# Sequence passes and a mean moved between two parts of up products, in a fused Fourier and two-MLP kernel on one core

## The chip, the cores and the metric

The kernel runs on one core of one Trainium2 chip. The metric is the device time of one execution in microseconds (us); the median of several executions is used. Engines are named as in the profile: PE is TensorE, DVE is VectorE, ACT is ScalarE, POOL is GpSimd, SP is SyncE (here it only issues DMAs).

## The reference

```python
def _attn_ref(x):                                   # x: 2 x 3008 x 256
    return np.fft.fft(np.fft.fft(x, axis=1), axis=2).real.astype(np.float32)

def _moe_ref(x, w_gate, w_val, w_out, rms_g):       # 6016 tokens, 256 -> 1536 -> 256
    rms = np.sqrt(np.mean(x * x, axis=-1, keepdims=True) + 1e-06)
    xn = x / rms * rms_g
    g = xn @ w_gate
    return ((g / (1.0 + np.exp(-g))) * (xn @ w_val) @ w_out).astype(np.float32)

def _moe2_ref(x, w_in, w_out):                      # 256 -> 2048 -> 256
    h = x @ w_in
    return (h * np.cos(h) @ w_out).astype(np.float32)

def reference(...):                                 # everything in float32
    return _moe2_ref(_moe_ref(_attn_ref(x).reshape(6016, 256), ...), ...)
```

## The kernel before

All arrays are fp32. The Fourier transform is done as matrix products in stages, and both MLPs work on tiles of columns.

**First stage** (lines 455 to 481). The sequence of 3008 is split as 32 x 94. `x` comes in 11 chunks, DVE folds each (L886 to L896), and PE multiplies it with a table (L474 to L479). 24 row pairs `m` form 8 groups of 3 (`GROUPS`), each with two products `c` = 0 and 1, in one of four PSUM banks `(2 * g + c) % 4`. ACT copies each bank out (L658) and turns two rows of `c` = 1 (L666); DVE does this for `c` = 1 of the last group (L906, L912), which PE computes first in its group. PE then waits for all of it (L482).

**Second stage**, the loop over `G` = 0 to 33 (L530 to L538): `features(G)` (PE L492), `pq_copy(G)` (DVE L925), `sequence(G)` (PE L508, L510), `uv_copy(p)` for two steps at a time (ACT L678). `square(q)` (ACT L694), `add_squares(q)` (POOL L1122), `rms(q)` (PE L526) and `mean_copy(q)` (ACT L703) make the mean squares in nine parts; `spread_mean(q)` (SP L349) sends them into `stat`, and `root` (ACT L711), `recip` (DVE L932) and `inverse` (POOL) make 1/rms for three groups of rows. Beside it the weights of the first up product are scaled and mixed on DVE (`SCALE_AT`, `MIX_AT`: the step `G` after which each piece is done; L942, L956) and each is split into a high and a low part: `split_w1(n)` on ACT (L717, L720), then `w1_add(n)` (POOL L1104), a DMA that adds in its destination, 512 KB each, six of them. Pieces 4 and 5 are split inside the first tile.

**Tiles** (6 of 502 columns). A product `three(...)` is three matmuls (L541, L542, L543). For each of 12 blocks `i`, `up1(t, i)` makes two halves `m` (gate and value), each with a sum part and a dif part in two PSUM banks. DVE makes `plus` from the sum part (L995) and two tokens from `plus` and the dif part (L1003, L1004; `g_ready` for the gate half, `v_ready` for the value half). ACT does Silu (L806), POOL the product with the value (L1184, token 1 first), ACT `h_hi` (L767), and `h_lo` comes from DVE for token 0 (L980) and from POOL for token 1 (L1095). `down(t, i)` follows two blocks behind. The second MLP follows in the same tile.

Each engine's instructions run in the order in which they are written. The parts that the change touches are ordered by hand. In the first tile SP runs this list, in order (a few lines between them left out):

```python
            for q in STAT_MEANS[2][:-1]:
                spread_mean(q)
            sp.wait_ge(uv_done, LAST)
            load(wo2_raw[:, :], wo2, wo2_in)
...
            for n in range(W1_CHUNKS):
                sp.wait_ge(w1_lo_done[n], 16)
            load(win2_raw[:, :], win2, win2_in)
            spread_mean(MEANS - 1)
```

The last part of the mean can therefore be spread only after all six `w1_add` have landed and `win2` (2 MB) has been issued. ACT's `root(1)` and `root(2)` stand in block `i` = 5 of the first tile, ahead of `hi1` of block 5.

Of the kernel before, what the change touches and what calls it, by code (L numbers as in the profile page):

```python
# [76 lines left out]
def build(nc, x, w1a, w1b, small, wo1, win2, wo2, t_seq1, t_feat, t_seq2, t_const, out):  # L77
    ctx = ExitStack()
    with ctx:
# [5 lines left out]
        def sb(name, shape, at, dt=F32):  # L85
# [94 lines left out]
        raw_a_in, raw_b_in = ([sem(f"raw_{ab}_in{i}") for i in range(3)] for ab in "ab")  # L180
        even_done, odd_done, folded, n1_done, n1_main, n1_last, n1_out, seq1_turned = (sem(n) for n in (
            "even_done", "odd_done", "folded", "n1_done", "n1_main", "n1_last", "n1_out", "seq1_turned"))
        pq_done, pq_out, uv_done, uv_main = (sem(n) for n in ("pq_done", "pq_out", "uv_done", "uv_main"))
# [265 lines left out]
        def _(pe):  # L449
# [8 lines left out]
            for g, ms in enumerate(GROUPS):  # L458
                for i, m in enumerate(ms):
                    if m in CHUNK_AT:  # L460
                        if m:
                            warm_up(2 if CHUNK_AT.index(m) < 4 else 0)
                        pe.wait_ge(folded, CHUNK_AT.index(m) + 1)
                        if CHUNK_AT.index(m) == HALF_FOLDED[0]:
                            pe.wait_ge(seq1_turned, 4)
                    for c in group_order(g):
                        if i == 0 and g >= 2:
                            pe.wait_ge(n1_out, 3 * (g - 2) + 2 * c + 1)
                        if m == 0 and c:
                            pe.wait_ge(seq1_turned, 2)  # L470
                        acc = ps[:, (2 * g + c) % 4, i * COLS1:(i + 1) * COLS1]
# [68 lines left out]
            def three(acc, w_hi, w_lo, v_hi, v_lo, start, stop):  # L540
                nc.tensor.matmul(acc, w_hi, v_hi, start=start, stop=False)  # L541
                nc.tensor.matmul(acc, w_hi, v_lo, start=False, stop=False)  # L542
                return nc.tensor.matmul(acc, w_lo, v_hi, start=False, stop=stop)  # L543

            def up1(t, j, halves=(0, 1)):

                for m in halves:
                    if j:
                        pe.wait_ge(plus_done, 2 * (C1 * t + j - 1) + m + 1)
                    elif not (isinstance(t, int) and t == 0):  # L550
                        pe.wait_ge(cos_done, 2 * (C2 * t - 1 + m))
                    if isinstance(t, int) and t == 0 and j % 4 == 0:
                        pe.wait_ge(w1_lo_done[j // 2 + m], 16)
                    w = slice(m * FF1 + j * P, m * FF1 + (j + 1) * P)
                    three(ps[:, bank_pair(m), 0:N], sum_hi[:, w], sum_lo[:, w],
                          uv_hi[:, 0, 0:N], uv_lo[:, 0, 0:N], True, True)
                    if j:
                        pe.wait_ge(v_ready if m else g_ready, (C1 - m) * t + j)
                    three(ps[:, bank_pair(m) + 1, 0:N], dif_hi[:, w], dif_lo[:, w],
                          uv_hi[:, 1, 0:N], uv_lo[:, 1, 0:N], True, True).then_inc(up_done, 1)  # L560

# [35 lines left out]
            def tile(t, first=False):  # L597
                if not first:
# [9 lines left out]
                up1(t, 1, halves=(1,))  # L608
                if not first:
                    down(t - 1, ITEMS - 1, tokens=(1,))  # L610
                for i in range(2, C1):
                    up1(t, i, halves=(0,))
# [33 lines left out]
        def _(act):  # L646
# [8 lines left out]
            for g, ms in enumerate(GROUPS):  # L655
                for c in range(1 if g == NG - 1 else 2):
                    act.wait_ge(n1_done, 2 * g + group_order(g).index(c) + 1)
                    nc.scalar.activation(  # L658
                        g_sb[:, :, c, :, 2 * ms[0]:2 * ms[-1] + 2],
                        ps[:, (2 * g + c) % 4, 0:len(ms) * COLS1].rearrange(  # L660
                            "p (n b k) -> p b k n", b=BATCH, k=2 * K1), ACT.Copy
                        ).then_inc(n1_main if c else n1_out, 1)
                    if c:
                        act.wait_ge(n1_main, g + 1)
                        for part in range(2):
                            nc.scalar.activation(  # L666
                                g_sb[0:1, :, 1, part::2, 2 * ms[0]:2 * ms[-1] + 2],
                                ps[0:1, (2 * g + 1) % 4, 1 - part:len(ms) * COLS1:2].rearrange(
                                    "p (n b k) -> p b k n", b=BATCH, k=K1), ACT.Copy,
# [125 lines left out]
            def tile(t, first=False, last=False):  # L795
                for i in range(C1):
# [6 lines left out]
                    elif not first:  # L803
# [75 lines left out]
        def _(dve):  # L879
            nc.vector.memset(zeros[:, :], 0.0).then_inc(zeros_ready, 1)  # L880
            nc.vector.memset(stat[0:1, 0, 0:1], 1.0).then_inc(root_ready, 1)
            for i in range(XL):
# [20 lines left out]
            nc.vector.tensor_scalar(w128[:, :], sm[:, 3:], g128, None, ALU.mult).then_inc(g_done, 1)  # L903
            dve.wait_ge(n1_done, 2 * NG - 1)
            ms = GROUPS[-1]
            nc.vector.tensor_copy(  # L906
                g_sb[:, :, 1, :, 2 * ms[0]:2 * ms[-1] + 2],
                ps[:, (2 * NG - 1) % 4, 0:len(ms) * COLS1].rearrange("p (n b k) -> p b k n", b=BATCH, k=2 * K1)
                ).then_inc(n1_last, 1)
            dve.wait_ge(n1_last, 1)  # L910
            for part in range(2):
                nc.vector.tensor_scalar(  # L912
                    g_sb[0:1, :, 1, part::2, 2 * ms[0]:2 * ms[-1] + 2],
                    ps[0:1, (2 * NG - 1) % 4, 1 - part:len(ms) * COLS1:2].rearrange(
                        "p (n b k) -> p b k n", b=BATCH, k=K1),
                    1.0 if part else -1.0, None, ALU.mult).then_inc(n1_out, 1)
            dve.wait_ge(g_done, 3)
# [175 lines left out]
        def _(pool):  # L1093
# [85 lines left out]
            def tile(t, first=False, last=False):  # L1179
                for i in range(C1 - 1):  # L1180
# [96 lines left out]
```

## Time and profile before

| what | value |
|---|---|
| median of 3 runs | 984.19 us (983.29 to 986.62) |
| the profiled execution: time | 984.3 us |
| the profiled execution: span, first to last instruction | 982.5 us |
| PE busy | 972.3 us (99% of the span) |
| DVE, ACT, POOL busy | 742.9, 638.7, 350.4 us |
| PE's waits for DVE at L541 (in tiles), together | 1.5 us (0.6 + 0.5 + 0.4) |
| granted PE clock | 1.000 of full |

The times of the text are microseconds from the start of the span. What lies around the span is 984.3 - 982.5 = 1.8 us. A matmul's duration in the profile is longer than the distance to the next, since they are pipelined: distances between starts are what counts on PE.

### The profile page before, as it was taken

Reading aid. Unit: us, or ns where it says so; the run is one execution under the profiler, and the core shown is the slowest. Engines: PE = TensorE matmul, PEld = TensorE weight load, DVE = VectorE, ACT = ScalarE, POOL = GpSimd, SP = SyncE. Lnnn points to the kernel's source line nnn. Section 1 sums busy time; section 2 is a strip of 40 time slices with the busy share of each in tenths; the row PEclk is TensorE's granted clock in tenths of the full one; section 3 lists DMA queues with packets and bytes.
Section 4 is the critical chain, followed back from the end, with each engine's and each line's share of the span. In section 5 each row is a group of like instructions: output and inputs, shape, how many; then the busy total and the mean of one; then the engine's idle time right before and its main releaser. Section 6 shows DMA issues by size and latency. Waiting matters only on the chain.

```text
span 982.5 us, 13009 instructions
## 1 busy us (share of the span) xinstructions
PE 972.3 (99%) x4518; PEld 807.9 (82%) x4518; DVE 742.9 (76%) x1028; ACT 638.7 (65%) x803; POOL 350.4 (36%) x292
## 2 busy tenths in 40 slices
PE   8999999999999999999999999999999999999998
PEld 8978788888888888888888888888888888888886
DVE  6887987768876768877667877767887767887665
ACT  5586778764468774458775448776448776437777
POOL 0377874027730007750007751005661004770000
PEclk9999999999999999999999999999999999999999
DMA  9788002001010001010001010001000000000001
GB/s 332 235 221 235 1 1 53 0 1 43 1 43 1 1 0 42 0 40 2 0 0 42 0 32 11 0 0 42 0 32 0 0 0 7 36 0 0 0 0 42
DMA packets 14082, 36.80 MB, mean 37 GB/s; under 512 B 2618, under 2 KB 6682, under 8 KB 13658
## 3 DMA queue, kind: packets, MB, share of 16 engines
q1 hardware_dynamic: 11978, 31.63, 9.4%
q0 software_dynamic: 2064, 4.72, 2.7%
q8 instruction: 15, 0.25, 0.1%
q14 instruction: 25, 0.20, 0.1%
HBM read 22.35 MB, written 9.26 MB: 32 GB/s over the span
## 4 chain that ended last, share of the span: by engine, by line
PE 91%; DMA 3%; POOL 2%; DVE 2%; issue 1%; ACT 1%; SPq 0%; DVEq 0%; ACTq 0%; POOLq 0%
PE ps L541 30%; PE ps L543 30%; PE ps L542 30%; DMA x_sb<-x 1%; POOL work L1184 1%; PE ps L492 1%; DMA stat<-mean_row 1%; DMA w_lo<-w_f 1%; PE ps L510 1%; PE ps L508 0%; SPq L319 0%; POOL squares L1122 0%; POOL uv_t L1141 0%; POOL w_lo L1104 0%; POOL h_lo L1095 0%
## 5 line engine op out<-in xcount | busy, mean ns | idle before, releaser
L541 PE MATMUL ps<-h_hi,wo_hi 128*128 128x502 f32 x672 | 261.5, 389 | 0.6 <-DVE h_lo L980 0.6
L543 PE MATMUL ps<-h_hi,wo_lo 128*128 128x502 f32 x672 | 261.3, 389 | 0.0
L542 PE MATMUL ps<-h_lo,wo_hi 128*128 128x502 f32 x672 | 261.1, 389 | 0.0
L1095 POOL TENSOR_TENSOR h_lo<-work,h_hi 128x502 fp32r<-128x502 f32 x92 | 101.5, 1111 | 373.8 <-ACT h_hi L782 369.9
L767 ACT ACTIVATE h_hi<-work 128x502 fp32r<-128x502 f32 x132 | 82.4, 626 | 174.2 <-POOL work L1184 173.9
L1082 DVE SCALAR_TENSOR_TENSOR work<-work,ps 128x1004 f32<-128x1004 f32 (+1 forms) x109 | 117.2, 1075 | 95.6 <-ACT work L864 95.2
L1068 DVE SCALAR_TENSOR_TENSOR work<-work,ps 128x1004 f32<-128x1004 f32 (+1 forms) x109 | 116.5, 1074 | 48.0 <-ACT work L850 47.9
L541 PE MATMUL ps<-x_hi,win_hi 128*128 128x502 f32 x384 | 150.0, 391 | 0.0
L541 PEld LDWEIGHTS ps<-h_hi,wo_hi 128*128 128x128 f32 x672 | 126.2, 188 | 28.2 <-issue 0.8
L542 PE MATMUL ps<-x_lo,win_hi 128*128 128x502 f32 x384 | 149.3, 389 | 0.0
L543 PE MATMUL ps<-x_hi,win_lo 128*128 128x502 f32 x384 | 149.2, 389 | 0.0
L543 PEld LDWEIGHTS ps<-h_hi,wo_lo 128*128 128x128 f32 x672 | 126.3, 188 | 25.9
L542 PEld LDWEIGHTS ps<-h_lo,wo_hi 128*128 128x128 f32 x672 | 126.3, 188 | 25.9
L995 DVE SCALAR_TENSOR_TENSOR plus<-u,w,ps 128x502 f32<-128x502 f32 x144 | 105.8, 735 | 50.6 <-PE ps L543 49.8
L850 ACT ACTIVATE work<-ps 128x1004 f32<-128x1004 f32 (+1 forms) x109 | 98.2, 907 | 60.1 <-PE ps L543 59.3
L859 ACT ACTIVATE work<-work 128x1004 f32<-128x1004 f32 (+1 forms) x109 | 102.7, 942 | 31.1 <-DVE work L1068 30.3
L1184 POOL TENSOR_TENSOR work<-work,uv_t 128x502 f32<-128x502 f32 x72 | 99.1, 1398 | 46.6 <-DVE uv_t L1004 44.8
L988 DVE TENSOR_TENSOR h_lo<-work,h_hi 128x502 fp32r<-128x502 f32 x172 | 114.3, 703 | 1.3
L541 PE MATMUL ps<-uv_hi,w_hi 128*128 128x502 f32 x288 | 112.8, 392 | 0.9 <-DVE work L1004 0.5
L542 PE MATMUL ps<-uv_lo,w_hi 128*128 128x502 f32 x288 | 112.0, 389 | 0.0
L543 PE MATMUL ps<-uv_hi,w_lo 128*128 128x502 f32 x288 | 111.9, 389 | 0.0
L782 ACT ACTIVATE h_hi<-work 128x1004 fp32r<-128x1004 f32 (+1 forms) x109 | 101.7, 939 | 14.8 <-PE ps L543 8.7
(89 smaller groups left out, 1275.7 us busy)
## 6 DMA issues: line engine op xcount, KB each, us to landing
out<-y_sb SPq DMA_DIRECT2D x10, 502.0 KB, 3.0
x_sb<-x SPq DMA_DIRECT2D x6, 768.0 KB, 10.3
w_lo<-w_f POOLq DMA_DIRECT2D x6, 512.0 KB, 7.0
uv_t<-uv_dram SPq DMA_DIRECT2D x6, 502.0 KB, 3.5
wo_raw<-wo SPq DMA_DIRECT2D x1, 2048.0 KB, 8.5
win_raw<-win SPq DMA_DIRECT2D x1, 2048.0 KB, 9.4
raw_b<-w1b SPq DMA_DIRECT2D x3, 512.0 KB, 12.4
raw_a<-w1a SPq DMA_DIRECT2D x3, 512.0 KB, 12.3
```

The source lines that it names most:

```text
L541: nc.tensor.matmul(acc, w_hi, v_hi, start=start, stop=False)
L542: nc.tensor.matmul(acc, w_hi, v_lo, start=False, stop=False)
L543: return nc.tensor.matmul(acc, w_lo, v_hi, start=False, stop=stop)
L782: nc.scalar.activation(h_hi[j % 2][:, gs, 0:N], work[j % 4][:, gs, :], ACT.Copy).then_inc(hi_done, gs.stop - gs.start)
L850: nc.scalar.activation(work[j % 4][:, gs, :], ps[:, bank_pair(j) + gs.start:bank_pair(j) + gs.stop, 0:N], ACT.Copy, bias=MAGIC).then_inc(r ...
L859: nc.scalar.activation(work[j % 4][:, gs, :], work[j % 4][:, gs, :], ACT.Sin, scale=TURN / 2).then_inc(sin_done, gs.stop - gs.start)
L988: nc.vector.tensor_tensor(h_lo[j % 2][:, g, 0:N], work[j % 4][:, g, :], h_hi[j % 2][:, g, 0:N].bitcast(F32), ALU.subtract).then_inc(hid_sp ...
L995: nc.vector.scalar_tensor_tensor(out=plus[m][:, :], in0=u128[:, :], scalar=w128[:, m * C1 + i:m * C1 + i + 1], in1=ps[:, bank_pair(m), 0:N ...
L1068: nc.vector.scalar_tensor_tensor(out=buf, in0=buf, scalar=MAGIC, in1=pair, op0=ALU.subtract, op1=ALU.subtract).then_inc(frac_done, gs.stop ...
L1082: nc.vector.scalar_tensor_tensor(out=buf, in0=buf, scalar=1.0, in1=pair, op0=ALU.subtract, op1=ALU.mult).then_inc(cos_done, gs.stop - gs.s ...
L1095: nc.gpsimd.tensor_tensor(dst, src, hi.bitcast(F32), ALU.subtract).then_inc(s, 1)
L1184: nc.gpsimd.tensor_tensor(work[i % 3][:, g, :], work[i % 3][:, g, :], value[i % 2][:, g, :], ALU.mult).then_inc(h_done[g], 1)
```

## The change

- First stage: six PSUM banks instead of four; the last group of three row pairs becomes a group of two and a group of one. DVE copies out `c` = 1 of both, with a semaphore of its own (`n1_turned`).
- `sequence(32)` and `sequence(33)` move from between the halves of `up1(0, 0)` to between the sum and dif parts of the halves of `up1(0, 1)`; `rms(7)` (the eighth mean) moves to between the sum and dif parts of `up1(0, 2)`'s first half. The last `uv_copy` on ACT moves behind the first Silu.
- `rms(6)` moves from step 32 to step 33. `square(8)` and `add_squares(8)` move from block 0 to block 1 of the first tile.
- The second `plus` buffer lies elsewhere, since `pq` is still read when it is first written.
- `w1_add(2)` moves ahead of `add_squares(5)` on POOL.
- The mixings of all weight pieces but the last are done by step 24, and the scalings by step 21.
- `down(0, 0)` takes token 1 first, and waits for the eighth mean's copy ahead of both tokens.

```diff
-        plus = [sb(f"plus{i}", [N], o_pq + i * TB // 2) for i in range(2)]
+        plus = [sb("plus0", [N], o_pq), sb("plus1", [N], o_x2 + 1024)]
-        GROUPS = [range(i, i + 3) for i in range(0, H // 2, 3)]
+        GROUPS = [range(i, i + 3) for i in range(0, H // 2 - 3, 3)] + [range(H // 2 - 3, H // 2 - 1), range(H // 2 - 1, H // 2)]
+        def n1_bank(g, c):
+            return (2 * g + c) % 6
         def group_order(g):
-            return (1, 0) if g == NG - 1 else (0, 1)
+            return (1, 0) if g >= NG - 2 else (0, 1)
-        RMS_AT = [8, 9, 15, 20, 24, 28, 32]
+        RMS_AT = [8, 9, 15, 20, 24, 28, 33]
-        SCALE_AT = [2, 6, 10, 19, 23, 28]
-        MIX_AT = [3, 5, 8, 9, 16, 18, 20, 22, 24, 26, 31, 32]
+        SCALE_AT = [2, 6, 10, 16, 20, 21]
+        MIX_AT = [3, 5, 8, 9, 11, 13, 18, 19, 23, 24, 31, 32]
-                        if i == 0 and g >= 2:
-                            pe.wait_ge(n1_out, 3 * (g - 2) + 2 * c + 1)
+                        if i == 0 and g >= 3:
+                            pe.wait_ge(n1_out, 3 * (g - 3) + 2 * c + 1)
-            pe.wait_ge(n1_out, 3 * NG)
+            pe.wait_ge(n1_out, 3 * NG - 4)
+            pe.wait_ge(n1_turned, 4)
...
-                up1(t, 1, halves=(0,))
                 if first:
+                    up1_sum(t, 1, 0)
+                    sequence(LAST - 2)
+                    up1_dif(t, 1, 0)
+                    up1_sum(t, 1, 1)
+                    sequence(LAST - 1)
+                    up1_dif(t, 1, 1)
+                    up1_sum(t, 2, 0)
                     rms(RMS_LATE[0])
+                    up1_dif(t, 2, 0)
                 else:
+                    up1(t, 1, halves=(0,))
                     down(t - 1, ITEMS - 1, tokens=(0,))
...
-                        down(t, 0, tokens=(0,))
                         pe.wait_ge(mean_out, MEANS - 1)
-                        down(t, 0, tokens=(1,))
+                        down(t, 0, tokens=(1, 0))
...
             up1(0, 0, halves=(0,))
-            sequence(LAST - 2)
-            sequence(LAST - 1)
+            pe.wait_ge(pq_out, LAST)
             pe.wait_ge(mean_out, len(RMS_AT))
             up1(0, 0, halves=(1,))
...
-            for p in range(LAST // 2):
+            for p in range(LAST // 2 - 1):
...
                     if first and i == 0:
+                        uv_copy(LAST // 2 - 1)
+                        mean_copy(RMS_LATE[0])
+                    if first and i == 1:
                         square(MEANS - 1)
-                        mean_copy(RMS_LATE[0])
...
             w1_add(1)
+            w1_add(2)
             add_squares(5)
             scale_uv(0)
             scale_u128(0)
-            w1_add(2)
             add_squares(6)
...
-                    if first and i == 0:
+                    if first and i == 1:
                         add_squares(MEANS - 1)
```

`up1` is otherwise cut into `up1_sum` and `up1_dif` with the same waits and matmuls, and DVE's copy of the last group becomes a loop over the last two groups.

## Rows read from the trace of the kernel before

**Rows 1.** Windows: busy us (instructions) of PE, PEld, DVE, ACT, POOL, then clock, DMA share, GB/s.
```profile
76.00:88.00 12.00, 12.00 (x62) 9.62 (x61) 9.51 (x16) 9.58 (x14) 10.84 (x11) 1.00 0.98 213
...
200.00:300.00 100.00, 100.00 (x443) 82.71 (x442) 78.59 (x117) 55.94 (x76) 51.43 (x41) 1.00 0.06 21
```
**Rows 2.** PE's waits in the whole span: total us, times, longest.
```profile
PE ps L526 <- POOL squares L1122: 1.3, 1, 1.3
...
PE ps L492 <- DVE g_sb L912: 0.9, 1, 0.9
PE ps L541 <- DVE h_lo L980: 0.6, 2, 0.4
```
**Rows 3.** The chain that ended last, 78 to 110: start, us, what.
```profile
78.28 7.38 DMA w_lo<-w_f
...
85.73 0.35 SPq L319
...
86.98 9.03 DMA stat<-mean_row
...
96.12 0.04 ACT stat L711
...
109.81 0.49 PE ps L541
```
**Rows 4.** Timeline, 24 to 26: start, duration, what.
```profile
24.56 0.58 DVE L906 COPY g_sb<-ps 128x408 f32<-128x408 f32 x1 [1.13 <-PE ps L475]
...
25.18 0.63 DVE L912 TENSOR_SCALAR g_sb<-ps 1x204 f32<-1x204 f32 x2
...
25.87 1.56 PE L492 MATMUL ps<-feat,g_sb 128*96 128x129 f32 x12 [0.88 <-DVE g_sb L912]
```
**Rows 5.** Timeline, 55 to 60.
```profile
55.20 0.81 ACT L694 ACTIVATE squares<-uv 128x752 f32<-128x752 f32 x1
55.33 1.21 DVE L935 TENSOR_TENSOR uv_lo<-uv_t,uv_hi 128x1004 fp32r<-128x1004 f32 x1 [0.25 <-ACT uv_hi L744]
...
56.15 1.29 POOL L1122 TENSOR_TENSOR squares<-squares 128x376 f32<-128x376 f32 x1
...
57.93 0.47 DVE L925 SCALAR_TENSOR_TENSOR pq<-feat,ps 96x256 f32<-96x256 f32 x1
...
59.18 0.47 PE L541 MATMUL ps<-uv_hi,w_hi 128*128 128x502 f32 x1
...
59.67 0.47 DVE L925 SCALAR_TENSOR_TENSOR pq<-feat,ps 96x256 f32<-96x256 f32 x1
```
**Rows 6.** ACT's timeline, 64 to 72.
```profile
64.73 0.98 ACT L694 ACTIVATE squares<-uv 128x940 f32<-128x940 f32 x1
65.61 0.22 ACT L703 ACTIVATE mean_row<-ps 128x94 f32<-128x94 f32 x1
66.69 0.62 ACT L767 ACTIVATE h_hi<-work 128x502 fp32r<-128x502 f32 x1 [0.85 <-POOL work L1184]
...
71.53 0.63 ACT L767 ACTIVATE h_hi<-work 128x502 fp32r<-128x502 f32 x1
```
**Rows 7.** POOL's timeline, 65 to 74.
```profile
65.33 2.49 POOL L1184 TENSOR_TENSOR work<-work,uv_t 128x502 f32<-128x502 f32 x2 [1.81 <-DVE uv_t L1004]
...
68.82 1.00 POOL L1122 TENSOR_TENSOR squares<-squares 128x470 f32<-128x470 f32 x1
...
72.68 1.08 POOL L1095 TENSOR_TENSOR h_lo<-work,h_hi 128x502 fp32r<-128x502 f32 x1
73.70 1.20 POOL L1104 DMA_DIRECT2D w_lo<-w_f  x1
```
**Rows 8.** DVE's and POOL's timelines: the same DVE instruction with and without POOL beside it.
```profile
74.25 0.68 DVE L980 TENSOR_TENSOR h_lo<-work,h_hi 128x502 fp32r<-128x502 f32 x1
...
114.31 1.25 DVE L980 TENSOR_TENSOR h_lo<-work,h_hi 128x502 fp32r<-128x502 f32 x1
...
113.72 1.30 POOL L1095 TENSOR_TENSOR win_lo<-win_raw,win_hi 128x512 fp32r<-128x512 f32 x1
```

More of the change, by code:

```diff
@@ L154, in build @@
         zeros = sb("zeros", [P], o_pq)
-        plus = [sb(f"plus{i}", [N], o_pq + i * TB // 2) for i in range(2)]
+        plus = [sb("plus0", [N], o_pq), sb("plus1", [N], o_x2 + 1024)]
+        assert o_work + 4 * GCOLS <= o_x2 + 1024 and o_x2 + 1024 + 4 * N <= o_hid - UVB
         o_end = o_pq + pad(max(TB, 16 * DIM))
@@ L180, in build @@
         raw_a_in, raw_b_in = ([sem(f"raw_{ab}_in{i}") for i in range(3)] for ab in "ab")
-        even_done, odd_done, folded, n1_done, n1_main, n1_last, n1_out, seq1_turned = (sem(n) for n in (
-            "even_done", "odd_done", "folded", "n1_done", "n1_main", "n1_last", "n1_out", "seq1_turned"))
+        even_done, odd_done, folded, n1_done, n1_main, n1_last, n1_turned, n1_out, seq1_turned = (sem(n) for n in (
+            "even_done", "odd_done", "folded", "n1_done", "n1_main", "n1_last", "n1_turned", "n1_out", "seq1_turned"))
         pq_done, pq_out, uv_done, uv_main = (sem(n) for n in ("pq_done", "pq_out", "uv_done", "uv_main"))
@@ L543, in three, with up1_sum, up1_dif @@
                 return nc.tensor.matmul(acc, w_lo, v_hi, start=False, stop=stop)
+            def up1_sum(t, j, m):
+                if j:
+                    pe.wait_ge(plus_done, 2 * (C1 * t + j - 1) + m + 1)
+                elif not (isinstance(t, int) and t == 0):
+                    pe.wait_ge(cos_done, 2 * (C2 * t - 1 + m))
+                if isinstance(t, int) and t == 0 and j % 4 == 0:
+                    pe.wait_ge(w1_lo_done[j // 2 + m], 16)
+                w = slice(m * FF1 + j * P, m * FF1 + (j + 1) * P)
+                three(ps[:, bank_pair(m), 0:N], sum_hi[:, w], sum_lo[:, w],
+                      uv_hi[:, 0, 0:N], uv_lo[:, 0, 0:N], True, True)
+            def up1_dif(t, j, m):
+                w = slice(m * FF1 + j * P, m * FF1 + (j + 1) * P)
+                if j:
+                    pe.wait_ge(v_ready if m else g_ready, (C1 - m) * t + j)
+                three(ps[:, bank_pair(m) + 1, 0:N], dif_hi[:, w], dif_lo[:, w],
+                      uv_hi[:, 1, 0:N], uv_lo[:, 1, 0:N], True, True).then_inc(up_done, 1)
             def up1(t, j, halves=(0, 1)):
                 for m in halves:
[L548 to L560, printed above, removed]
+                    up1_sum(t, j, m)
+                    up1_dif(t, j, m)
             def up2(t, j):
@@ L602, in tile @@
                     up1(t, 0, halves=(1,))
-                up1(t, 1, halves=(0,))
                 if first:
+                    up1_sum(t, 1, 0)
[5 more added lines that the diff above has]
+                    up1_sum(t, 2, 0)
                     rms(RMS_LATE[0])
+                    up1_dif(t, 2, 0)
                 else:
+                    up1(t, 1, halves=(0,))
                     down(t - 1, ITEMS - 1, tokens=(0,))
-                up1(t, 1, halves=(1,))
-                if not first:
+                    up1(t, 1, halves=(1,))
                     down(t - 1, ITEMS - 1, tokens=(1,))
+                    up1(t, 2, halves=(0,))
                 for i in range(2, C1):
-                    up1(t, i, halves=(0,))
+                    if i > 2:
+                        up1(t, i, halves=(0,))
                     if first and i == LAST_MEAN_AT + 1:
@@ L655, in _ @@
             for g, ms in enumerate(GROUPS):
-                for c in range(1 if g == NG - 1 else 2):
+                for c in range(1 if g >= NG - 2 else 2):
                     act.wait_ge(n1_done, 2 * g + group_order(g).index(c) + 1)
@@ L659, in _ @@
                         g_sb[:, :, c, :, 2 * ms[0]:2 * ms[-1] + 2],
-                        ps[:, (2 * g + c) % 4, 0:len(ms) * COLS1].rearrange(
+                        ps[:, n1_bank(g, c), 0:len(ms) * COLS1].rearrange(
                             "p (n b k) -> p b k n", b=BATCH, k=2 * K1), ACT.Copy
@@ L667, in _ @@
                                 g_sb[0:1, :, 1, part::2, 2 * ms[0]:2 * ms[-1] + 2],
-                                ps[0:1, (2 * g + 1) % 4, 1 - part:len(ms) * COLS1:2].rearrange(
+                                ps[0:1, n1_bank(g, 1), 1 - part:len(ms) * COLS1:2].rearrange(
                                     "p (n b k) -> p b k n", b=BATCH, k=K1), ACT.Copy,
@@ L903, in _ @@
             nc.vector.tensor_scalar(w128[:, :], sm[:, 3:], g128, None, ALU.mult).then_inc(g_done, 1)
[L904 to L916, printed above, removed]
+            for g in (NG - 2, NG - 1):
+                ms, bank = GROUPS[g], n1_bank(g, 1)
+                dve.wait_ge(n1_done, 2 * g + 1)
+                nc.vector.tensor_copy(
+                    g_sb[:, :, 1, :, 2 * ms[0]:2 * ms[-1] + 2],
+                    ps[:, bank, 0:len(ms) * COLS1].rearrange("p (n b k) -> p b k n", b=BATCH, k=2 * K1)
+                    ).then_inc(n1_last, 1)
+                dve.wait_ge(n1_last, g - NG + 3)
+                for part in range(2):
+                    nc.vector.tensor_scalar(
+                        g_sb[0:1, :, 1, part::2, 2 * ms[0]:2 * ms[-1] + 2],
+                        ps[0:1, bank, 1 - part:len(ms) * COLS1:2].rearrange(
+                            "p (n b k) -> p b k n", b=BATCH, k=K1),
+                        1.0 if part else -1.0, None, ALU.mult).then_inc(n1_turned, 1)
             dve.wait_ge(g_done, 3)
```

2 lines of the change are left out of this document (1 added, 1 removed).

## The prediction

> **What bounds the kernel now.** The windows come first: from 200 to 300 us, and in every window after it up to 960, PE is busy all the time at a granted clock of 1.00, the 2.4 GHz level [rows 1], and the change adds no PE work, so a gain or a loss can only come from the stretch before, where PE waits. PE's waits name the places: 1.3 us on POOL's squares ahead of `rms(6)`, 0.9 us on DVE's last copy of the first stage, 0.6 us on `h_lo` in two pieces, at `down(0, 0)` and, near 98 us, at `down(0, 5)` [rows 2]. I then read the chain that ended last, and it decides the case. Read it backwards from 109.81, where PE's last wait of the head ends: to `root(2)` on ACT at 96.12; to the DMA of the ninth mean into `stat`, issued at 86.98 and 9.03 us on its way; to the load of `win2` just ahead of it on SP's queue, at 85.73; to the last of the six weight adds, `w1_add(5)`, issued by POOL at 78.28 and landed after 7.38 us [rows 3]. SP's list says why: `win2` waits for all six. From 109.81 on PE doesn't wait for anything that matters. So the end of the kernel moves by as much as `w1_add(5)` moves, if its landing and what follows last as long as now. What PE gains before 78 us is not yet a gain: it arrives earlier at `down(0, 5)` and waits there longer.
>
> **First stage.** Before, the tail behind the last product is one copy of 408 columns (0.58 us) and two turns of 204 (0.63 together), and PE starts at 25.87 [rows 4]. After, the tail is 136 columns and turns of 68. By those two rows (0.58 for 408, 0.31 for 204: 0.0013 us a column) these take 0.22 and twice 0.14, 0.50 in all. The larger group's tail (272 columns 0.40, turns of 136 0.45) runs on DVE's idle time of 1.13 us before [rows 4], but can begin only some 0.75 before L906 did, at 23.8, and ends at 24.7, 0.15 after the last product. 25.87 - (24.7 + 0.5 + 0.05) is 0.6; small copies rarely come out as cheap as a line through two rows says, so I take 0.35, with bounds 0 and 0.6. The six banks cost nothing and by themselves give nothing: no row shows PE waiting for ACT's copies; they keep the group of one from waiting for a bank. Steps 0 to 31 are paced by PE, so the 0.35 goes through to everything at 56 us. Times below leave it out, and it comes into the sum at the end.
>
> **`rms(6)` a step later, `w1_add(2)` earlier.** PE loses 1.3 us at 57.55 [rows 2]. `features(33)` and `sequence(30)` (0.9 us, half of the steady 0.87 each and the switch) now run in it. Does `add_squares(6)` also come earlier, with the DMA issue gone ahead of it? Its input `square(6)` ends at 56.01 (55.20 + 0.81), and DVE's `uv_lo`, which reads two operands from SBUF, runs to 56.54 [rows 5]. DVE's `h_lo` takes 0.68 us alone and 1.25 when it is issued at 114.31, inside POOL's instruction from 113.72 to 115.02: it ends 0.54 after POOL [rows 8]. So the one waits for the other: the squares, 0.85 us by themselves (1.29 less what `uv_lo` holds them), still end at 57.4, and `rms(6)` starts at 57.5; if they did not wait it would be 57.0. The Trainium skill, SBUF — State Buffer, "SBUF: two separate sides", calls the port pair of the two engines an exclusive lock that the first holds for its whole instruction when DVE reads two inputs from SBUF; that too would give 57.5, and this trace agrees with 1.25 against 0.68 us. PE gains 0.9 of the 1.3. `w1_add(2)` fits into the wait that POOL had before `add_squares(5)` (2.6 us) and costs nothing. The mixings go to steps where DVE waits for PE; two stay at steps 31 and 32.
>
> **Into the tile.** DVE is next. `up1(0, 0)` waits for `pq_copy(32)`, which ends at 57.93 + 0.47 = 58.40 [rows 5]: it starts at 58.45, against 59.18 before, 0.73 earlier. The other half waits for `pq_copy(33)`, 60.14, which is a new wait of 0.3 on PE. DVE then runs through `plus` and tokens without a wait, since two sequence passes (0.8 us) no longer stand between. The first value is ready, and POOL's first product starts, at 64.4 against 65.33 [rows 7]: 0.94 earlier. PE's own gain at `down(0, 0)` comes to 1.45, as its three waits on DVE there shrink too.
>
> **What is queued behind the moved passes.** ACT now does `uv_copy(16)` and `mean_copy(7)` behind the first Silu, ahead of `hi1(0)`. PE reaches `rms(7)` after `up1(0, 0)` second half (60.2 + 1.44), two sums and two difs at 0.68 each with a switch (3.0), two sequence passes (0.84) and one more sum (0.68): 66.1. The copy follows half a us later, and `h_hi` starts at 66.75, against 66.69 [rows 6], although the product was ready at 65.65. The gain of 0.94 is gone for token 1 of block 0. ACT's second Silu comes 0.6 earlier than before; `square(8)`, 0.88 in distance [rows 6], now stands behind it, then the two splits: `h_hi` of block 1 at 71.7 against 71.53 [rows 6].
> POOL's `h_lo` of block 1 then runs at 72.4 against 72.68 (there it waited for the product), and behind it comes the moved `add_squares(8)` of 1.0 us [rows 7], ahead of `w1_add(4)`. DVE's `h_lo` (0.68) waits for the same lock since 73.0 and may go first: another 0.55. `w1_add(4)` goes out at 73.4 + 1.0 = 74.4, or 74.95, against 73.70 [rows 7]: 0.7 or 1.25 later. The squares are no new work, but before they ran from 68.82, and there POOL would now wait for ACT's Silu (until 68.9) anyway. From `w1_add(4)` to `w1_add(5)` is 78.28 - 73.70 = 4.58, one product, one `h_lo` and the issue, as before.
>
> **The sum.** `w1_add(5)` moves by +0.7 to +1.25 less the first stage's 0.35: +0.35 to +0.9. I take +0.6, the middle, since nothing tells which of the two gets the lock. The chain behind it is unchanged. The profiled execution took 984.3; 984.3 + 0.6 = 984.9. The median shown is 0.1 under the profiled execution: 984.8.
>
> **Free edits.** The second `plus` buffer's home: written and read by DVE alone as before; in `x2_hi`, which ACT writes only after the last token of the first MLP is made. Token 1 first in `down(0, 0)`: POOL's `h_lo` (68.4) is there before DVE's (69.1), PE arrives at 69.05, so it hides a wait of 0.1 to 1 us, which is PE's time and is given back at 98 us. The loop over tiles 1 to 5 keeps its order. A new wait: `up1(0, 4)`'s second half waits for the ninth mean's copy, on ACT behind the fourth Silu, perhaps 0.7 us; PE's again, and covered by the same later wait.
>
> **Rivals.**
> *POOL runs through early (22%).* If `rms(7)` and the squares cost POOL nothing, all of its list from 65.33 to 78.28, in which it never idles, moves by 0.94 + 0.35 = 1.3 earlier: 983.0 in the profiled execution, 982.9. It needs `rms(7)` half a us or more before my 66.1 and products faster than in rows 7. For it: POOL's total work there is the same. Against: ACT's order, worked out above.
> *PE's gain stays (7%).* If the chain over `win2` had slack that I don't see, PE keeps 0.35 + 1.45 and part of the late waits: 984.3 - 1.8 - 0.7, near 981.7. Against: the chain is unbroken from 78.28 to 109.81 [rows 3].
> *Slower: the transfers slip (13%).* SP spreads the eighth mean before it issues `wo2` (2 MB) and the 1.4 MB of `uv`. That mean is copied 1.0 later, 0.65 with the first stage, and the DMA engines are 98% busy in 76 to 88 [rows 1]. If the backlog moves by the full 0.65, the adds 4 and 5 land behind it: with the upper 0.9 for their issue and a first stage that gives nothing (0.35), 0.65 + 0.9 + 0.35 = 1.9: 986.1. It decides once `w1_add(5)` lands later than 87. The Trainium skill, DMA: Bandwidth & Descriptors, "Queues, rings and completion order", has a semaphore increment land only after every earlier write of that DMA engine, across its queues: a reason why a mean of 1.5 KB needs 9.03 us [rows 3], and the adds would wait for late stores in the same way.
> *As forecast (58%):* 984.1 to 985.6, no difference that can be told.
>
> **Range and chances.** About 0.3% (3 us) is what a measurement can tell here. 982.7 to 986.5 holds the forecast, most of the early rival, and most of the late one; outside lie the kept gain, and single mishaps. All of PE's waits that could go are 0.9 + 1.3 [rows 2] and the 1.5 in the tiles (the table above), 3.7 us, so over 0.3% faster needs nearly all of them: 4%. Over 0.3% slower needs the late rival and a us more: 4%. Within: 92%.
>
> **What the new profile would show.** PE's first feature matmul at 25.5; PE's wait for the squares under 0.5 us and a new one ahead of the second half of `up1(0, 0)`; POOL's first product at about 64; `mean_row`'s copy at 66.3 just ahead of `h_hi`; `w1_add(4)` at 74.1 to 74.6 and `w1_add(5)` at 78.6 to 79.2; `root(2)` at 96.5 to 97; and PE's wait for `h_lo` near 98, 0.2 before, grown to 1.5 or more. The prediction is wrong if `w1_add(5)` is issued before 78, if its landing or that of the mean isn't near 7.4 and 9.0, or if PE no longer waits at 98.

## The result and the profile after

The changed kernel takes 987.26 us (median of 21, 985.61 to 992.3), the kernel before 984.96 us (median of 21, 983.29 to 988.9): ratio 1.0028, interval 1.0017 to 1.0039. It is slower by 2.3 us in the medians and 2.8 by the ratio, just under the 0.3% that I had called the limit of what can be told, and outside my range. The profiled execution took 986.18 us, its span 984.2 us: it was one of the faster ones, 0.9 us under the median of the 13 executions at a mean granted clock of 1.00 (987.08), so the profile shows less of the loss than the times do.

PE's waits of the changed kernel, in total us, times, longest (`rms` is now L531, a product L546 to L548, `h_lo` on DVE L1001):

```profile
PE ps L546 <- DVE h_lo L1001: 1.5, 1, 1.5
PE ps L531 <- issue: 1.5, 1, 1.5
...
PE ps L546 <- ACT mean_row L721: 0.8, 1, 0.8
PE ps L497 <- ACT g_sb L676: 0.5, 1, 0.5
```

Against [rows 2]: the wait of 1.3 us for the seventh mean's squares is gone, and 1.5 us stand at another mean. The wait for `h_lo` has grown from 0.2 near 98 us (0.6 in two pieces) to 1.5, and the ninth mean's copy costs 0.8. The chain that ended last (start, us, what), the counterpart of [rows 3]:

```profile
79.72 6.88 DMA w_lo<-w_f
86.67 0.35 SPq L323
...
88.29 9.42 DMA stat<-mean_row
...
98.11 0.62 ACT h_hi L785 x2
...
111.51 0.50 PE ps L546
```

It is the same chain, 1.70 us later where PE leaves it (111.51 against 109.81), and the span is 1.7 us longer. The sixth weight add goes out 1.44 later (79.72 against 78.28); its landing is 0.5 quicker; from the load of `win2` to `root(2)` it is 0.75 longer (86.67 to 97.81, against 85.73 to 96.12).

Where the new wait comes from is seen on POOL, DVE and PE of the changed kernel (timelines; L1143 is `add_squares`, L1125 `w1_add`, L1150 to L1156 `inverse(0)`, L977 a mixing, L963 a scaling, L953 the reciprocal):

```profile
38.01 1.28 POOL L1143 TENSOR_TENSOR squares<-squares 128x376 f32<-128x376 f32 x1 [3.88 <-ACT squares L712]
39.24 2.92 POOL L1125 DMA_DIRECT2D w_lo<-w_f  x1
40.98 1.26 POOL L1150 TENSOR_TENSOR stat<-stat 6x94 f32<-6x94 f32 x1
42.31 0.48 POOL L1152 TENSOR_TENSOR stat<-stat 6x94 f32<-6x94 f32 x1
42.89 1.48 POOL L1154 TENSOR_SCALAR stat<-stat 6x94 f32<-6x94 f32 x1
44.45 0.86 POOL L1156 TENSOR_TENSOR stat<-stat 6x94 f32<-6x94 f32 x1
45.27 1.48 POOL L1143 TENSOR_TENSOR squares<-squares 128x376 f32<-128x376 f32 x2
...
38.57 1.28 DVE L977 SCALAR_TENSOR_TENSOR w_f<-raw_a,gvec,raw_b 128x512 f32<-128x512 f32 x1
...
40.16 0.72 DVE L953 RECIPROCAL stat<-stat 6x94 f32<-6x94 f32 x1
...
45.42 1.62 DVE L963 TENSOR_SCALAR raw_b<-raw_b,gvec 128x512 f32<-128x512 f32 x1
...
44.33 0.39 PE L515 MATMUL ps<-seq,pq 96*128 96x94 f32 x2
46.21 0.37 PE L531 MATMUL ps<-squares,consts 128*32 128x94 f32 x8 [1.50 <-issue]
```

The mixing at step 13 (0.74 by itself) and POOL's squares (0.84 in the kernel before) meet and take 1.28 each. The reciprocal of step 14 and `inverse(0)` follow late, and each small operation of `inverse(0)` is longer too (1.26, 0.48, 1.48 and 0.86 us, against 1.01, 0.34, 0.72 and 0.34 before). The squares of the fourth mean, next on POOL, start only at 45.27 (before: 42.81), and PE waits for them from 44.7 to 46.21.

### The profile page after: what moved, and what is told of

It reads as the page before. It is cut to its first block, busy times and chain, and to the rows that moved or that the text cites. A ratio compares the mean times of both kernels' runs of the same rounds, so it can differ in the third digit from the quotient of the medians.

```text
span 984.2 us, 13014 instructions
## 1 busy us (share of the span) xinstructions
PE 972.4 (99%) x4518; PEld 808.9 (82%) x4518; DVE 743.5 (76%) x1031; ACT 638.6 (65%) x804; POOL 352.5 (36%) x292
## 4 chain that ended last, share of the span: by engine, by line
PE 93%; DMA 3%; DVE 1%; ACT 1%; POOL 1%; issue 1%; SPq 0%; DVEq 0%; ACTq 0%
PE ps L546 30%; PE ps L547 30%; PE ps L548 30%; PE ps L497 2%; DMA x_sb<-x 1%; DMA stat<-mean_row 1%; PE ps L515 1%; DMA w_lo<-w_f 1%; PE ps L513 1%; POOL work L1205 0%; SPq L323 0%; ACT h_hi L785 0%; DVE x_sb L906 0%; PE ps L482 0%; PE ps L531 0%
## 5 line engine op out<-in xcount | busy, mean ns | idle before, releaser
L546 PE MATMUL ps<-h_hi,wo_hi 128*128 128x502 f32 x672 | 261.7, 389 | 1.5 <-DVE h_lo L1001 1.5
L548 PE MATMUL ps<-h_hi,wo_lo 128*128 128x502 f32 x672 | 261.6, 389 | 0.0
L546 PE MATMUL ps<-x_hi,win_hi 128*128 128x502 f32 x384 | 150.2, 391 | 0.0
L546 PEld LDWEIGHTS ps<-h_hi,wo_hi 128*128 128x128 f32 x672 | 126.3, 188 | 28.5 <-DVE h_lo L1001 2.2
L548 PE MATMUL ps<-x_hi,win_lo 128*128 128x502 f32 x384 | 149.4, 389 | 0.0
L548 PEld LDWEIGHTS ps<-h_hi,wo_lo 128*128 128x128 f32 x672 | 126.4, 188 | 25.8
L546 PE MATMUL ps<-uv_hi,w_hi 128*128 128x502 f32 x288 | 113.0, 392 | 1.5 <-ACT mean_row L721 0.8
L548 PE MATMUL ps<-uv_hi,w_lo 128*128 128x502 f32 x288 | 112.1, 389 | 0.0
## 6 DMA issues: line engine op xcount, KB each, us to landing
x_sb<-x SPq DMA_DIRECT2D x6, 768.0 KB, 10.4
```

## The experiments

Each was measured beside the kernel before. "Add 5 of 6" and "6 of 6" are the issue of the last two `w1_add`, and `root(2)` and the end of the span are given from PE's first feature matmul, since the loading of `x` shifts that by about 1 us between executions of like kernels (25.87 to 26.86 with the old first stage, 24.93 to 26.21 with the new). What the first stage itself gives is therefore not in these columns. "Early" is a `root(2)` that runs right behind `root(1)`, before 92.4 in the span.

| kernel | ratio (95%) | add 5, 6 of 6 | root(2) | span end |
|---|---|---|---|---|
| before | 1 | 47.83, 52.41 | 70.25 | 956.63 |
| changed | 1.0028 (1.0017 to 1.0039) | 49.76, 54.07 | 72.16 | 958.55 |
| a1 old mix steps | 1.0029 (1.0015 to 1.0042) | 52.05, 56.36 | 74.44 | 960.87 |
| a2 only mix steps | 1.0024 (1.0014 to 1.0035) | 49.15, 53.71 | 71.44 | 957.89 |
| a3 one mix moved back | 1.0017 (1.0009 to 1.0026) | 49.23, 53.52 | 71.75 | 958.23 |
| a4 mean before win2 | 0.9996 (0.9985 to 1.0007) | 49.85, 54.15 | early | 955.99 |
| b1 mixings apart | 1.0011 (1.0002 to 1.0020) | 49.12, 53.43 | 71.65 | 958.06 |
| b2 before, mean first | 0.9998 (0.9984 to 1.0013) | 47.86, 52.43 | early | 955.84 |
| b3 apart, mean first | 0.9992 (0.9982 to 1.0003) | 49.13, 53.43 | early | 955.24 |
| b4 apart, squares back | 0.9996 (0.9987 to 1.0005) | 46.86, 51.15 | 69.26 | 955.72 |
| c1 changed again | 1.0038 (1.0024 to 1.0051) | 51.75, 56.04 | 74.12 | 960.49 |
| c2 apart, squares back, mean first | 0.9971 (0.9961 to 0.9982) | 47.73, 52.02 | early | 953.94 |
| c3 also scaling early | 0.9973 (0.9963 to 0.9984) | 47.75, 52.04 | early | 954.03 |
| c4 before, squares later | 1.0025 (1.0015 to 1.0034) | 49.49, 53.80 | 71.98 | 958.35 |
| d1 changed, squares back | 1.0013 (1.0001 to 1.0025) | 50.35, 54.66 | 72.98 | 959.34 |
| d2 before, squares later, mean first | 0.9999 (0.9989 to 1.0008) | 49.48, 53.80 | early | 955.66 |

The first two rows are the two kernels of the first series. In every kernel in which the mean comes after `win2`, the end of the span less `root(2)` is 886.4 us (886.36 to 886.48). A kernel in which `root(2)` comes 1.7 later ends 1.7 later. With the mean first, `root(2)` no longer waits, and the end is PE's own.

**a1: the old steps for scaling and mixing, in the changed kernel.**

```diff
-        SCALE_AT = [2, 6, 10, 16, 20, 21]
-        MIX_AT = [3, 5, 8, 9, 11, 13, 18, 19, 23, 24, 31, 32]
+        SCALE_AT = [2, 6, 10, 19, 23, 28]
+        MIX_AT = [3, 5, 8, 9, 16, 18, 20, 22, 24, 26, 31, 32]
```

> The changed kernel with the scaling and mixing steps of before; all else as changed. Theory A (mixings at steps 11 to 19 stand beside POOL's squares and inverse(0), so that the squares for the fourth mean come late, PE waits 1.5 us at 44.7, and POOL's list carries it to the last weight add): the wait at 44.7 is gone, the last weight add is issued at 78.2 to 79.0 instead of 79.7, and the ratio to before falls from 1.0028 to 0.9995 to 1.0010. Theory B (what I predicted: the moved squares and ACT's order behind the moved passes are the cost, the mixings are free): the ratio stays at 1.002 to 1.003.

Measured 1.0029, outside theory A's range and inside theory B's; the last add goes out at 81.29 in the span, later than theory A had it. The wait at 44.7 is gone, and another of 2.2 us is there, from 52.7 to 54.89. Timelines of DVE and POOL, and windows of all engines (busy us of PE, PEld, DVE, ACT, POOL, then granted clock, DMA share, GB/s), of this kernel:

```profile
50.12 4.32 DVE L977 SCALAR_TENSOR_TENSOR w_f<-raw_a,gvec,raw_b 128x512 f32<-128x512 f32 x1
...
49.40 1.05 POOL L1143 TENSOR_TENSOR squares<-squares 128x376 f32<-128x376 f32 x1
50.22 2.47 POOL L1162 TENSOR_TENSOR uv_t<-uv_t,inv_t 128x502 f32<-128x502 f32 x2
52.45 1.43 POOL L1167 TENSOR_TENSOR u<-u,inv_t 128x502 f32<-128x502 f32 x1
```

The windows:

```profile
53.00:54.00 1.00, 0.00 (x0) 0.00 (x0) 1.00 (x1) 1.00 (x2) 0.88 (x1) 1.00 1.14 211
...
56.00:57.00 1.00, 1.00 (x7) 1.00 (x6) 0.41 (x2) 0.62 (x2) 0.40 (x1) 0.50 0.93 346
57.00:58.00 1.00, 1.00 (x6) 1.00 (x6) 1.00 (x2) 0.00 (x0) 0.00 (x0) 0.50 1.10 240
```

The mixing of step 26 is issued at 50.12, while POOL's squares run; three POOL products follow these without a gap, to 53.88, and the mixing ends at 54.44, 0.56 after them: it ran only when POOL had nothing more. The same place in the kernel before:

```profile
50.37 0.84 POOL L1122 TENSOR_TENSOR squares<-squares 128x376 f32<-128x376 f32 x1 [2.61 <-ACT squares L694]
51.19 3.04 POOL L1141 TENSOR_TENSOR uv_t<-uv_t,inv_t 128x502 f32<-128x502 f32 x2
...
51.09 0.74 DVE L956 SCALAR_TENSOR_TENSOR w_f<-raw_a,gvec,raw_b 128x512 f32<-128x512 f32 x1
```

Here the mixing was issued 0.1 before the end of the same squares, ran between them and the first product, and took 0.74, while the two products took 3.04 instead of 2.47. Counted from the first feature matmul, the mixing is issued at the same time in both (25.19 and 25.22), and POOL's operations follow each other without a gap in both. What differs is that in a1 the squares stand right behind the issue of the moved `w1_add(2)` and end 0.2 later (25.52 against 25.34). That this made the mixing lose its turn is likely, but no run shows it by itself. Either way the old steps are no longer free once the rest of the change is there: undoing this part alone exchanges one collision for another, so the ratio of 1.0029 is no support for theory B.

PE is idle during its wait, and then its granted clock is 0.50 for some 3 us, of which more under c1. Of a1's seven executions four have a mean granted clock of 0.998; the three at 1.00 have a median of 985.37, 1.0 us over before's 984.39, so much of a1's ratio is the clock.

**a2: the new steps alone, in the kernel before** (the diff of a1 the other way).

> The kernel before with the new scaling and mixing steps alone. Theory A: a wait of PE of about 1 to 1.5 us appears near 44.9, and the kernel is slower than before by 1 to 2.5 us, ratio 1.0010 to 1.0025. Theory B: ratio 0.9995 to 1.0005, no new wait.

Measured 1.0024, two waits of PE for squares, 2.5 us together, the longer one 1.5: theory A. That the mixings cost nothing, as I had it, is refuted.

**a3: one mixing from step 13 to 16, in the changed kernel.**

```diff
-        MIX_AT = [3, 5, 8, 9, 11, 13, 18, 19, 23, 24, 31, 32]
+        MIX_AT = [3, 5, 8, 9, 11, 16, 18, 19, 23, 24, 31, 32]
```

> The changed kernel with one single mixing moved, from step 13 to step 16 (where before had one); the others stay at the new steps. Theory A in its narrow form (the mixing at step 13, 38.6, delays the reciprocal at step 14 and the second weight piece, and these inverse(0) on POOL): reciprocal at 39.1 instead of 40.2, PE's wait at 44.7 under 0.6 us, ratio to before 0.9998 to 1.0015. Theory A in its wide form (all of the early mixings together): the wait stays over 1 us and the ratio over 1.0018. Theory B: no change from 1.0028.

Measured 1.0017. The wait for the fourth mean is gone and the reciprocal starts at 39.42: the narrow form, as far as the wait goes. The ratio lies between the two forms (1.0015 at most, over 1.0018), and its interval takes in both.

**a4: the last mean spread before `win2`, in the changed kernel.**

```diff
+            spread_mean(MEANS - 1)
             for n in range(W1_CHUNKS):
                 sp.wait_ge(w1_lo_done[n], 16)
             load(win2_raw[:, :], win2, win2_in)
-            spread_mean(MEANS - 1)
```

> The changed kernel with SP's order changed: the last mean is spread before the wait for the six weight adds and the load of win2, instead of behind it. Theory A2 (the end of the head is set by the chain last weight add, win2, last mean, root on ACT): root(2) comes at about 91 instead of 97.8, PE's wait of 1.5 us for h_lo near 100 goes, and the time falls by 1.5 to 2.5 us from the changed kernel, ratio to before 1.0000 to 1.0012. Rival (PE's time lost at 44.7 is lost for good and the late chain only hides it): the ratio stays over 1.0022.

Measured 0.9996, a little better than forecast: the loss is gone, with PE's wait of 1.5 us near 44.7 still in place. The late chain does set the end, as predicted.

**b1: mixings apart, in the changed kernel.**

```diff
-        SCALE_AT = [2, 6, 10, 16, 20, 21]
-        MIX_AT = [3, 5, 8, 9, 11, 13, 18, 19, 23, 24, 31, 32]
+        SCALE_AT = [2, 6, 10, 19, 21, 28]
+        MIX_AT = [3, 5, 8, 9, 16, 18, 20, 22, 23, 24, 31, 32]
```

> The changed kernel with mixings at 16, 18, 20, 22, 23, 24 (four of them where before had them) and scalings at 19, 21, 28: none stands beside inverse(0) at steps 11 to 15, and all but the last pair are done before POOL's unbroken run of uv and u128 products from 50. Theory A, as the first four runs leave it (it is the meeting of one DVE mixing with POOL's two-input instructions that costs, in either of two places): no wait of PE at 44 to 46 and no mixing over 1.7 us, last weight add issued at 78.3 to 79.2, root(2) at 96.3 to 97.2, ratio to before 1.0000 to 1.0010. Rival (the rest of the change, the squares and ACT's order in the first tile, carries most of the loss): last weight add after 79.4, ratio over 1.0015.

Measured 1.0011, just over the forecast and under the rival's 1.0015. POOL of this kernel, against the fence of the changed one above:

```profile
38.20 0.85 POOL L1143 TENSOR_TENSOR squares<-squares 128x376 f32<-128x376 f32 x1 [3.88 <-ACT squares L712]
38.99 2.05 POOL L1125 DMA_DIRECT2D w_lo<-w_f  x1
40.10 1.02 POOL L1150 TENSOR_TENSOR stat<-stat 6x94 f32<-6x94 f32 x1
...
41.63 0.72 POOL L1154 TENSOR_SCALAR stat<-stat 6x94 f32<-6x94 f32 x1
...
42.75 0.84 POOL L1143 TENSOR_TENSOR squares<-squares 128x376 f32<-128x376 f32 x1
```

The squares are back at 0.85 us and those of the fourth mean 2.5 us earlier. Add 6 of 6 is at 79.27 in the span, just over the forecast of this run, `root(2)` at 97.49, 0.3 over it. One collision is left: the scaling of step 28, issued at 52.76 beside the products that a1 showed, takes 2.34 us, where others take 0.47.

**b2, b3: the mean first, in the kernel before and in b1's.** The edit is that of a4.

> The kernel before with the last mean spread ahead of the wait for the weight adds and of win2. Theory A2 (the late chain sets the end of before too, by as much as PE waits at 98 and 107 to 110, 0.9 us in all): root(2) before 92, those waits gone, ratio to before 0.9988 to 0.9996. Rival (the chain was not binding in before): ratio 0.9997 to 1.0003.

> Both edits in the changed kernel: mixings apart, and the last mean ahead of win2. If PE's gain in the first tile is real and only hidden by the late chain, it now shows: 0.2 from the first stage, about 1 us from rms(6) and the passes, 0.9 from the late waits: ratio to before 0.9975 to 0.9988, the fastest of all. If the moved passes give PE nothing, ratio 0.9990 to 1.0000, as the kernel before with the mean first.

Measured 0.9998 and 0.9992. From the first feature the span is 0.8 and 1.4 us shorter than before, as expected of b2 and at the low end of b3, and the medians say the same (983.83 and 983.05 against 984.58). But both ratios lie in the ranges of the rivals, and their intervals reach into both ranges, so the times settle neither.

**b4: b1 with the squares back in block 0.**

```diff
                     if first and i == 0:
                         uv_copy(LAST // 2 - 1)
+                        square(MEANS - 1)
                         mean_copy(RMS_LATE[0])
-                    if first and i == 1:
-                        square(MEANS - 1)
...
-                    if first and i == 1:
+                    if first and i == 0:
                         add_squares(MEANS - 1)
```

> As the run with the mixings apart, but square(8) and add_squares(8) back in block 0 of the first tile, where before had them. My predicted mechanism (the squares of 1 us, and up to 0.55 of DVE's, ahead of the fifth weight add): the fifth weight add goes out 0.5 to 1.2 us earlier than with the mixings apart alone, and the ratio falls by 0.0005 to 0.0012. Rival (ACT, not POOL's squares, paces block 1: in block 0 square(8) stands in the time in which ACT waits for the eighth mean, but add_squares then delays POOL's next product): under 0.3 us of change.

Measured 0.9996 against 1.0011 of b1 (same chip, same runs of before). Add 5 of 6 goes out 2.26 us earlier, more than the 0.5 to 1.2 expected: not only the squares, but ACT's `square(8)` leaves block 1.

**c1: the changed kernel again.**

> The changed kernel itself once more, beside the kernel before on one chip, as a control for the three next to it. Theory A: the same profile as the first one, PE's wait of 1.5 us ahead of the fourth mean, ratio 1.002 to 1.003; and if the longer wait is what sometimes brings PE's granted clock down for some us, more of its executions than of before show a mean clock of 0.998. Rival (the gap to the mixings-apart run came from the chip and not from the wait): ratio 1.001 to 1.0015 here, and no difference in the clocks.

Measured 1.0038, over the forecast of 1.002 to 1.003. Three of five executions are at a mean granted clock of 0.998 (7 of 21 in the first series; the kernel before 3 of 21 beside c1, none of 11 in b1 and in b4, none of 8 in c2). This time the profiled one was among them. Its windows, columns as above:

```profile
44.00:46.00 2.00, 1.07 (x10) 0.91 (x9) 2.00 (x5) 1.11 (x3) 1.92 (x3) 1.00 1.03 177
46.00:47.00 1.00, 0.43 (x9) 0.32 (x10) 1.00 (x1) 0.00 (x0) 1.00 (x2) 1.00 0.12 21
47.00:48.00 1.00, 1.00 (x7) 1.00 (x8) 0.64 (x2) 0.00 (x0) 0.97 (x2) 0.62 0.62 60
48.00:49.00 1.00, 1.00 (x7) 1.00 (x7) 0.64 (x2) 0.38 (x1) 0.00 (x0) 0.50 0.84 275
49.00:50.00 1.00, 1.00 (x7) 1.00 (x7) 0.48 (x1) 1.00 (x3) 0.00 (x0) 0.50 1.04 308
50.00:51.00 1.00, 1.00 (x8) 1.00 (x8) 0.04 (x1) 0.97 (x2) 0.00 (x0) 0.68 0.93 141
51.00:52.00 1.00, 1.00 (x11) 1.00 (x10) 1.00 (x2) 0.81 (x3) 0.42 (x1) 1.00 1.13 228
```

PE stands still for 1.5 us in 44 to 47. Then the granted clock goes from 1.00 (2.4 GHz) to 0.50 (1.2 GHz), and is back at 1.00 from 51 on. The windows' clocks lack 0.38 + 0.5 + 0.5 + 0.32 = 1.7 us of full clock, and POOL's first product comes 1.8 us later after the first feature than in the first profile of the same kernel (41.45 against 39.63). The profiles of a1 and d1, which have 2.2 and 1.5 us of wait in front, show the same. The first profile of the changed kernel and that of a2 have the same wait of 1.5 us and no fall.

**c2, c3: what the change can give.** c2 is b4's kernel with a4's edit. c3 also has `SCALE_AT = [2, 6, 10, 17, 19, 21]`.

> Mixings apart, squares back in block 0, and the last mean spread ahead of win2: what PE gains in the first tile can no longer be hidden by the late chain. If the moved passes and the rms step are worth what PE's timeline says, ratio 0.9978 to 0.9990; if another chain takes over (the landing of win2 or the second MLP's weights), a new wait of PE after 100 us and a ratio of 0.9990 or more.

> As the run before, with the scalings at 17, 19, 21 instead of 19, 21, 28: the one at step 28 took 2.35 us instead of 0.47 beside POOL's unbroken run of products in the run with the mean first. It should take 0.47 again, features and sequences of steps 28 to 31 lose their 0.2 to 0.5 us of waits, and the time falls by 0.2 to 0.6 us more; the cost, if one is seen, is a backlog of DVE of up to 1 us at steps 22 to 24, which PE has two steps of slack for.

Measured 0.9971 and 0.9973, 981.84 and 981.87 us against 984.45: faster than both kernels. What is left of PE's waits in c2 after the first stage:

```profile
PE ps L531 <- issue: 0.3, 1, 0.3
PE ps L546 <- DVE work L1024: 0.2, 1, 0.2
PE ps L497 <- DVE pq L945: 0.2, 1, 0.2
```

Both are better than the forecast of c2. c3's further 0.2 to 0.6 us did not come: its waits for squares are 0.7 us, in two, instead of 0.3. The new one is again at the fourth mean, where the last operation of `inverse(0)` on POOL takes 1.64 us instead of 0.34.

**c4: the squares alone, in block 1 of the kernel before** (b4's edit the other way).

> The kernel before with one edit of the change alone: square(8) and add_squares(8) in block 1 instead of block 0. My predicted mechanism: the fifth and the sixth weight add go out 0.7 to 1.3 us later, root(2) with them, ratio 1.0007 to 1.0015. Rival (in the kernel before POOL would use the freed time of block 0, so the move is neutral there): the adds move by under 0.3 us, ratio 0.9997 to 1.0003.

Measured 1.0025, more than expected: 2.2 us by the executions at a granted clock of 1.00, 1.7 in the profile. POOL and ACT of this kernel, the counterpart of [rows 6, 7]:

```profile
73.20 1.08 POOL L1096 TENSOR_TENSOR h_lo<-work,h_hi 128x502 fp32r<-128x502 f32 x1 [0.87 <-ACT h_hi L767]
74.24 1.46 POOL L1123 TENSOR_TENSOR squares<-squares 128x470 f32<-128x470 f32 x1
75.64 1.20 POOL L1105 DMA_DIRECT2D w_lo<-w_f  x1
...
69.60 0.97 ACT L694 ACTIVATE squares<-uv 128x940 f32<-128x940 f32 x1
70.48 1.05 ACT L717 ACTIVATE w_hi<-w_f 128x1024 fp32r<-128x1024 f32 x1
71.56 1.06 ACT L720 ACTIVATE w_lo<-w_hi 128x1024 fp32r<-128x1024 f32 x1
72.52 1.12 ACT L767 ACTIVATE h_hi<-work 128x502 fp32r<-128x502 f32 x2
```

`square(8)` stands ahead of the two splits and of `h_hi` on ACT, POOL waits 0.87 for `h_hi`, and then has the squares at 1.46 (0.97 from start to start in [rows 7]; the rest is DVE's `h_lo`) ahead of the weight add, which goes out 1.66 later than before.

**d1, d2: the other half of the division, and the squares without the chain.** d1 is the changed kernel with b4's edit; d2 is c4's kernel with a4's.

> The changed kernel with square(8) and add_squares(8) back in block 0, all else as changed, the early mixings too. If the squares carry most of the loss through the weight adds: the fifth weight add goes out near 47.5 after the first feature matmul (49.76 in the changed kernel, 47.83 before), root(2) at 70.0 to 70.8 (72.16 and 70.25), and the ratio falls to 1.0000 to 1.0014; what is left over 1.0000 is the early mixings' wait at 44.7 and what the clock does after it. If the early mixings carry most: ratio stays over 1.0020.

> The kernel before with the squares in block 1 (alone 1.0025) and with the last mean spread ahead of win2. If the squares cost only by the chain over the weight adds, win2 and the last mean, they are now free: ratio as with the mean first alone, 0.9985 to 1.0003. If they cost PE by another way as well, ratio over 1.0012.

Measured 1.0013 and 0.9999. d1's profile was one with the clock down after the wait, so its add at 50.35 isn't comparable; its time is inside the forecast. d2's is that of b2: the squares cost nothing once the mean doesn't wait for the weight adds.

## Why the prediction was wrong

With the executions at a granted clock of 1.00 alone, each median against that of before beside it, the mixings and the squares divide the loss like this:

| | mixings apart | mixings as changed |
|---|---|---|
| squares in block 0 | -0.3 us (b4) | +1.5 us (d1) |
| squares in block 1 | +1.3 us (b1) | +2.8 us (c1) |

c1 has only two such executions. The first series has 13, and their median of 987.08 is 2.1 us over that of all executions of before (984.96; their clocks aren't on record), so the 2.8 may be too high by up to 0.7.

1. **What bounds the kernel: right.** The end moves with `root(2)`, to 0.1 us, in all kernels that keep SP's order; a4 and d2 cut the chain, and the loss goes.
2. **PE's gains are hidden by it: right in kind, the forecast wait hit by luck.** PE's wait at `down(0, 5)` grew to 1.5 us, as forecast, but not for the reason given. The lines, before and after:

```profile
98.78 0.50 PE L541 MATMUL ps<-h_hi,wo_hi 128*128 128x502 f32 x1 [0.20 <-DVE h_lo L980]
...
100.48 0.49 PE L546 MATMUL ps<-h_hi,wo_hi 128*128 128x502 f32 x1 [1.53 <-DVE h_lo L1001]
```

PE comes to this wait at 98.58 before and at 98.95 after. I had it 1.8 us earlier; it is 0.4 later, and the wait is long because `root(2)` is 1.7 later. The gain is there where neither the mixings nor the squares take it away: in b4 PE comes 2.0 us earlier after the first feature (70.70 against 72.71), and c2, which also removes what hides it, is 0.29% faster than before.
3. **First stage: right.** From the start of the last pass of the last product to the first feature matmul it is 1.28 us before (24.59 to 25.87) and 0.94 after (24.71 to 25.65): 0.34 for my 0.35. The view puts the end of the wait down to ACT's copy of 136 columns, which ends at 25.42; DVE's last turn, which PE waits for too, ends at 25.55, so DVE's tail may still be what counts.
4. **`rms(6)` and the first tile: right in the main, seen in b1, where the mixings cost PE no wait.** Its wait is 0.3 us, the first product at 38.83 after the first feature, 0.63 earlier than before (0.94 forecast; the missing 0.3 is not explained), the mean's copy at 66.81 just ahead of `h_hi`, the last weight add 1.02 later after the first feature: my +0.7 to +1.25. DVE's `h_lo` did get the port ahead of the squares (1.46). The wait of 0.3 us forecast ahead of the second half of `up1(0, 0)` did not come. No run takes `rms(6)`, the moved passes or the first stage by itself, so what each of them gives is not shown.
5. **The step that failed: "the mixings go to steps where DVE waits for PE".** I put their cost at nothing by looking at DVE alone, in the very paragraph that shows that a DVE operation with two SBUF inputs and a POOL operation wait for each other. At steps 11 to 19 they stand beside POOL's squares, a weight add's issue and `inverse(0)`. Alone in the kernel before that costs 1.3 us at full clock (a2, four executions), in the changed kernel 1.5 to 1.8 by the table, or 0.8 with the first series in place of c1. In the executions in which the clock falls, 1 to 2 us come on top. None of my rivals had it. The profile of the changed kernel has only 0.5 us of it at `root(2)` (72.16 against 71.65 in b1), since that execution was a fast one.
6. **A term mis-sized: "the chain behind it is unchanged".** I took +0.6 for `w1_add(5)` less the first stage. In b1 that term came out at +1.0 in the span, and the chain behind it at another +0.4 (landing 0.5 quicker, `win2` to `root(2)` 0.9 longer). The six kernels with the squares in block 1 and the mean behind `win2` take 10.9 to 11.6 from its load to `root(2)`, the four with them in block 0 take 9.8 to 10.4 (b4 and before). Together that is b1's 1.4 at `root(2)` and 1.3 in the time, for my 0.6 (0.9 at most). Alone in the kernel before (c4) the moved squares cost 1.7 in the profile, where the last weight add has moved by 1.4. What lengthens the rest is open. Part of it is SP's two issues of the mean: they take 1.73 to 1.89 us in the six kernels, 1.21 to 1.52 in the four, and no run tried that by itself.
7. **Two slips on the way, without effect on the forecast.** In the sum of the late rival a first stage that gives nothing was given back to the adds, but not to the mean (0.65 should be 1.0), so its 1.9 is 2.25. And the 0.68 us of DVE's `h_lo` in [rows 8] is not one without POOL beside it: POOL's products are issued at 74.49, within it, and it is they that wait (2.96 us for the two, against 2.49 in [rows 7]).

## What to carry to other kernels

A free slot on one engine isn't free if the operation put there shares a port with what runs beside it on another: lay out both engines' timelines before moving it, and ask what each of the two is followed by. When every PE gain vanishes, look for the chain that the gains run into. Here one line moved in SP's list took more off the changed kernel (1.0028 to 0.9996, a4) than the change had cost, though only 0.8 us off the kernel before (b2); with it and two pieces undone the change saved 0.29% (c2). An undone part can meet something that the rest has moved: a1 would have acquitted the mixings if its trace had not been read.

## What the runs showed of the hardware

- A DVE mixing of 0.74 us took 4.32 when it was issued during one POOL operation and three more followed without a gap (a1). In other places DVE came in between two POOL operations: `h_lo` at 73.58 in the changed kernel, 1.01 us, and POOL's squares after it 1.46. The Trainium skill, SBUF — State Buffer, "SBUF: two separate sides", has the loser blocked until the winner's instruction ends; the traces agree for one instruction, and add that the loser may be passed over again. What decides it, no run here shows.
- A DVE scaling with one tensor read from SBUF (0.47 us in other places) took 2.34 us beside POOL's products (b1).
- After a PE wait of 1.5 us the granted clock fell from the 2.4 GHz to the 1.2 GHz level for some 3.4 us in a part of the executions only (profiles of c1 and d1, and of a1 after 2.2 us; not in those of the changed kernel and a2). In c1 that cost 1.7 us, as much again as the wait.
